# Attention and two dense layers on one core: TensorE's operations grouped by kind within a slot, and an order of their own for the first five slots

## The reference

```python
scores = scale * np.matmul(q, k.transpose(0, 1, 3, 2))     # q, k, v: 2 x 8 heads x 576 x 64
kth = np.partition(scores, -32, axis=-1)[..., -32:-31]
scores = np.where(scores >= kth, scores, -1e9)
attn = exp(scores - max) / (sum + 1e-9)
x = matmul(attn, v)                                        # as 1152 rows x 512
x = ((x @ w_a) * (x @ w_b)) @ w_out                        # 512 -> 1536 -> 512
p = domain_probs / (domain_probs.sum(-1) + 1e-9)
out = sum over e of p[:, e] * (relu(x @ w1[e]) @ w2[e])    # 4 experts, 512 -> 1024 -> 512
```

## Time and profile before

| | |
|---|---|
| time, median of 3 runs (lowest, highest) | 848.16 us (845.84, 848.91) |
| the profiled execution | 849.11 us, span 847.3 us |
| mean granted clock | 0.972 |
| busy: PE, PEld, DVE, ACT, POOL | 807.8, 713.1, 457.9, 384.6, 297.1 us |
| instructions | 13113 |

### The profile page before, as it was taken

How to read it: one execution, slowest core, us unless ns; L and a number is a source line. 1 busy time by engine, 2 the same in 40 slices (tenths; PEclk the granted TensorE clock), 3 DMA queues, 4 the chain that set the end, 5 groups by cost and what they waited for, 6 DMA issues and landing times.

```text
span 847.3 us, 13113 instructions
## 1 busy us (share of the span) xinstructions
PE 807.8 (95%) x4985; PEld 713.1 (84%) x4985; DVE 457.9 (54%) x902; ACT 384.6 (45%) x712; POOL 297.1 (35%) x269
## 2 busy tenths in 40 slices
PE   4468999999999999999999999999999999999998
PEld 3346788888888888888889899899899898898996
DVE  5979999899999999998124112122121121221121
ACT  5665787777777777777444011311032010230110
POOL 3766875454545454545331000530016000440000
PEclk9557999999999999999999999999999999999999
DMA  9540685456545654445688500230004100000000
GB/s 233 160 117 1 219 242 206 150 193 200 187 148 183 254 170 158 163 155 173 209 285 300 219 1 1 99 100 1 1 1 141 58 1 1 1 1 38 14 25 38
DMA packets 71631, 102.59 MB, mean 121 GB/s; under 512 B 32528, under 2 KB 48912, under 8 KB 71568
## 3 DMA queue, kind: packets, MB, share of 16 engines
q1 hardware_dynamic: 70512, 101.48, 36.6%
q10 hardware_dynamic: 1056, 0.26, 0.2%
HBM read 88.36 MB, written 13.37 MB: 120 GB/s over the span
## 4 chain that ended last, share of the span: by engine, by line
PE 88%; ACT 4%; POOL 4%; issue 2%; DMA 1%; DVE 1%; SPq 0%; ACTq 0%; POOLq 0%
PE ps L612 24%; PE ps L632 23%; PE ps L522 16%; PE ps L507 8%; PE ps L471 5%; PE ps L442 5%; PE ps L451 4%; PE ps L480 1%; POOL p_sb L1007 1%; ACT p_sb L702 1%; POOL wa_lo L1041 1%; DMA wo<-wo_d 1%; PE ps L402 1%; ACT pT L709 1%; PE ps L514 0%
## 5 line engine op out<-in xcount | busy, mean ns | idle before, releaser
L769 ACT ACTIVATE h_hi<-ps 128x384 fp32r<-128x384 f32 x96 | 47.0, 491 | 269.7 <-PE ps L612 269.5
L874 DVE MAX8 m<-work 128x8 f32<-128x576 f32 x216 | 152.3, 747 | 0.0
L1057 POOL TENSOR_TENSOR w_lo<-w_raw,w_hi 128x2048 fp32r<-128x2048 f32 x12 | 55.1, 4617 | 244.5 <-ACT w_hi L765 244.5
L933 DVE SCALAR_TENSOR_TENSOR h_lo<-ps,h_hi 128x384 fp32r<-128x384 f32 x96 | 53.3, 557 | 156.8 <-ACT h_hi L769 156.8
L612 PE MATMUL ps<-x_hi,w_hi 128*128 128x384 f32 x384 | 129.0, 336 | 0.0
L612 PE MATMUL ps<-x_hi,w_lo 128*128 128x384 f32 x384 | 128.8, 336 | 0.0
L612 PE MATMUL ps<-x_lo,w_hi 128*128 128x384 f32 x384 | 128.8, 335 | 0.0
L632 PE MATMUL ps<-w_hi,h_hi 128*128 128x512 f32 x288 | 112.2, 390 | 0.0
L632 PE MATMUL ps<-w_hi,h_lo 128*128 128x512 f32 x288 | 112.2, 390 | 0.0
L632 PE MATMUL ps<-w_lo,h_hi 128*128 128x512 f32 x288 | 112.1, 389 | 0.0
L880 DVE MATCH_REPLACE8 work<-m,work 128x576 f32<-128x576 f32 x144 | 106.0, 743 | 0.0
(11 more groups left out here) (90 smaller groups left out, 1507.8 us busy)
## 6 DMA issues: line engine op xcount, KB each, us to landing
wo<-wo_d SPq DMA_DIRECT2D x96, 512.0 KB, 4.9
w_raw<-moe_w_in SPq DMA_DIRECT2D x16, 1024.0 KB, 6.6
wo_d<-wo SPq DMA_DIRECT2D x12, 512.0 KB, 4.5
w_raw<-moe_w_a_in SPq DMA_DIRECT2D x4, 768.0 KB, 6.0
w_raw<-moe_w_b_in SPq DMA_DIRECT2D x4, 768.0 KB, 5.5
wo_raw<-moe_w_out_in SPq DMA_DIRECT2D x12, 256.0 KB, 3.9
v_sb<-v_in SPq DMA_DIRECT2D x18, 128.0 KB, 3.8
x_d<-x_hi_out SPq DMA_DIRECT2D x9, 256.0 KB, 3.0
```

What stands on the lines that cost most here:

```text
L769: copy(h_hi[:, m, :], ps[:, UP + m % FREE_UP, 0:GN], ACT.Relu).then_inc(ac_r, 1)
L874: nc.vector.max(m8[:, par, i, 8 * r:8 * r + 8], work[:, i, :]).then_inc(ve_top, 1)
L933: nc.vector.scalar_tensor_tensor(h_lo[:, m, :], ps[:, UP + m % FREE_UP, 0:GN], 0.0, h_hi[:, m, :].bitcast(F32), ALU.max, ALU.subtract).the ...
L1057: nc.gpsimd.tensor_tensor(lo[:, s, :], raw[s][:], hi[:, s, :].bitcast(F32), ALU.subtract).then_inc(done, 1)
```

## The change

TensorE's order in slots 5 to 40 becomes: scores, send, up(wa), y_transpose, h_transpose, p_transpose, up(wb), q_transpose, inv_spread, keys, weighted_sum. inv_transpose stands between the two heads of p_transpose and writes a part of bank 3 instead of ps_a; the waits on `ac_a` and `ac_i` that went with ps_a go. Slots 0 to 4 have a function `first_slot`: p_transpose, q_transpose, scores of pair n + 2, weighted_sum, inv_spread. (The scores of pair 1 are still made in slot 0, and slot 4 makes none.)

ScalarE: x_hi moves between the two below_tops, y_out between the two exponentials, and p_out with inv_turned moves from behind the copy of a to ahead of slice_hi and chunk_hi. VectorE: sums after 1 pass instead of 2; for tile 0, sums after pass 10 of pair 4 (was 8), scale and x_low after passes 2 and 4 of pair 5 (were 4 and 6).

```diff
--- before.py
+++ after.py
@@ -443,8 +443,11 @@
                                                   kT[rows, b, pr, cols], start=True, stop=True)
                 mm.then_inc(pe_s, 1)
 
-            def p_transpose(n):
+            def p_transpose(n, t):
                 for head in range(2):
+                    if head and t is not None:
+                        pe.wait_ge(ac_s, 2 * min(n + 2, NP - 1) + head + 1)
+                        inv_transpose(t)
                     pe.wait_ge(ac_e, 2 * n + head + 1)
                     pe.wait_ge(ac_s, 2 * min(n + 2, NP - 1) + head + 1)
                     for c in range(KC):
@@ -482,7 +485,7 @@
 
             def inv_transpose(t):
                 pe.wait_ge(ve_den, 2 * t + 2)
-                nc.tensor.transpose(ps_a[:, 0:P], x_inv[:].rearrange("p r h -> p (r h)"), ident[:]).then_inc(pe_i, 1)
+                nc.tensor.transpose(ps[:, 3, P:2 * P], x_inv[:].rearrange("p r h -> p (r h)"), ident[:]).then_inc(pe_i, 1)
 
             def inv_spread(t):
                 pe.wait_ge(ac_i, 2 * t + 1)
@@ -536,7 +539,25 @@
             q_transpose(range(1, PR), ps_x)
             for pr in range(1, PR):
                 keys_pair(0, pr)
-            for n in range(LAST + 1):
+            def first_slot(n):
+                if n == 0:
+                    scores(1)
+                else:
+                    p_transpose(n - 1, scaled_tile(n + 1))
+                if next_q(n) is not None:
+                    pe.wait_ge(ld_q, 16 + 32 * next_q(n))
+                    q_transpose(range(PR), ps_a)
+                if n < LAG_AB - 1:
+                    scores(n + 2)
+                if n:
+                    weighted_sum(n - 1)
+                if scaled_tile(n + 1) is not None:
+                    pe.wait_ge(po_pick, PR + 1)
+                    inv_spread(scaled_tile(n + 1))
+
+            for n in range(LAG_AB):
+                first_slot(n)
+            for n in range(LAG_AB, LAST + 1):
                 m, u = unit_of(n), turned_unit(n)
                 if scaled_tile(n) is not None:
                     pe.wait_ge(ac_i, 2 * scaled_tile(n) + 2)
@@ -546,41 +567,30 @@
                     scores(n + 1)
                 if sent_of(n) is not None:
                     send(sent_of(n))
+                if m < PR:
+                    pe.wait_ge(po_w, SLICES.index((0, m)) + 1)
+                if m % PR == 0:
+                    pe.wait_ge(ve_xT, m // PR + 1)
+                pe.wait_ge(ac_a, m)
+                pe.wait_ge(ac_q, min((n + 1) // PR + 2, NT + 1))
+                up(wa_hi, wa_lo, ps_a, m, pe_a)
+                if finished_tile(n) is not None:
+                    y_transpose(finished_tile(n))
                 if u is not None:
                     h_transpose(u)
-                if m is not None:
-                    if m < PR:
-                        pe.wait_ge(po_w, SLICES.index((0, m)) + 1)
-                    if m % PR == 0:
-                        pe.wait_ge(ve_xT, m // PR + 1)
-                    pe.wait_ge(ac_a, m)
-                    if n % PR == 1:
-                        pe.wait_ge(ac_i, 2 * min(n // PR, NT))
-                    pe.wait_ge(ac_q, min((n + 1) // PR + 2, NT + 1))
-                    up(wa_hi, wa_lo, ps_a, m, pe_a)
-                if finished_tile(n) is not None:
-                    y_transpose(finished_tile(n))
                 if pair_of(n) is not None:
-                    p_transpose(pair_of(n))
-                if scaled_tile(n + 1) is not None:
-                    if m is not None:
-                        pe.wait_ge(ac_a, m + 1)
-                    inv_transpose(scaled_tile(n + 1))
-                if m is not None:
-                    if m < PR:
-                        pe.wait_ge(po_w, SLICES.index((1, m)) + 1)
-                    pe.wait_ge(ac_b, m)
-                    if u is not None:
-                        pe.wait_ge(ac_h, 2 * u + 2)
-                    up(wb_hi, wb_lo, ps_b, m, pe_b)
+                    p_transpose(pair_of(n), scaled_tile(n + 1))
+                if m < PR:
+                    pe.wait_ge(po_w, SLICES.index((1, m)) + 1)
+                pe.wait_ge(ac_b, m)
+                if u is not None:
+                    pe.wait_ge(ac_h, 2 * u + 2)
+                up(wb_hi, wb_lo, ps_b, m, pe_b)
                 if next_q(n) is not None:
-                    if m is not None:
-                        pe.wait_ge(ac_a, m + 1)
+                    pe.wait_ge(ac_a, m + 1)
                     pe.wait_ge(ld_q, 16 + 32 * next_q(n))
                     q_transpose(range(PR), ps_a)
                 if scaled_tile(n + 1) is not None:
-                    if n == PR:
-                        pe.wait_ge(po_pick, PR + 1)
                     pe.wait_ge(ac_pT, 2 * pair_of(n) + 2)
                     inv_spread(scaled_tile(n + 1))
                 if n in KEYS1:
@@ -711,7 +721,7 @@
 
             def inv_turned(t):
                 act.wait_ge(pe_i, 2 * t + 1)
-                copy(invT[:], ps_a[:, 0:P], ACT.Copy).then_inc(ac_i, 1)
+                copy(invT[:], ps[:, 3, P:2 * P], ACT.Copy).then_inc(ac_i, 1)
 
             def inv_out(t):
                 act.wait_ge(pe_i, 2 * t + 2)
@@ -783,24 +793,30 @@
                 j, m, u = pair_of(n), unit_of(n), turned_unit(n)
                 if j is not None:
                     below_top(j, 0)
+                if scaled_tile(n) is not None:
+                    x_hi(scaled_tile(n))
+                if j is not None:
                     below_top(j, 1)
                 if n + 1 < NP:
                     scores_out(n + 1, 0)
-                if scaled_tile(n) is not None:
-                    x_hi(scaled_tile(n))
                 if j is not None:
                     exponentials(j, 0)
+                if finished_tile(n) is not None:
+                    y_out(finished_tile(n))
+                if j is not None:
                     exponentials(j, 1)
                 if n + 1 < NP:
                     scores_out(n + 1, 1)
-                if finished_tile(n) is not None:
-                    y_out(finished_tile(n))
                 if u is not None:
                     h_out(u)
                 if n in (NP + 2, NP + 3):
                     act.wait_ge(pe_x, NP)
                     act.wait_ge(pe_s, NP)
                     expert_hi(0, n - NP - 2, 0)
+                if j is not None:
+                    p_out(j)
+                if scaled_tile(n + 1) is not None:
+                    inv_turned(scaled_tile(n + 1))
                 for i in HIGH_IN.get(n, ()):
                     slice_hi(i)
                 for g in CHUNKS_IN.get(n, ()):
@@ -809,10 +825,6 @@
                     act.wait_ge(pe_a, m + 1)
                     act.wait_ge(po_h, m)
                     copy(a_sb[:], ps_a[:, 0:FS], ACT.Copy).then_inc(ac_a, 1)
-                if j is not None:
-                    p_out(j)
-                if scaled_tile(n + 1) is not None:
-                    inv_turned(scaled_tile(n + 1))
                 if finished_tile(n) is not None:
                     x2_out(finished_tile(n))
                 if m is not None:
@@ -862,7 +874,7 @@
                 for i in range(2):
                     dve.wait_ge(ac_s, 2 * n + i + 1)
                     nc.vector.max(m8[:, par, i, 0:8], s_sb[:, ring[i], :]).then_inc(ve_top, 1)
-                between(n, 2)
+                    between(n, 1 + i)
                 for i in range(2):
                     dve.wait_ge(ve_top, base + i + 1)
                     nc.vector.match_replace(work[:, i, :], m8[:, par, i, 0:8], s_sb[:, ring[i], :], LOWEST).then_inc(ve_top, 1)
@@ -907,8 +919,8 @@
                 nc.vector.tensor_tensor(xT_lo[:, t % 2, :, :], xu[:].rearrange("p (c t) -> p c t", c=DK),
                                         xT_hi[:, t % 2, :, :].bitcast(F32), ALU.subtract).then_inc(ve_xT, 1)
 
-            SUMS, SCALE, LOW = 2, 10, 11
-            FIRST_SUMS, FIRST_SCALE, FIRST_LOW = 8, 4, 6
+            SUMS, SCALE, LOW = 1, 10, 11
+            FIRST_SUMS, FIRST_SCALE, FIRST_LOW = 10, 2, 4
 
             def between(n, done):
                 t = scaled_tile(n)
```

## The result

The changed kernel takes 856.85 us (median of 4 runs, 856.14 to 857.28), the kernel before 847.25 in the same comparison (845.84 to 848.91): ratio 1.0121, 95% interval 1.0100 to 1.0141. It is 9.6 us slower. The profiled execution took 857.28 us with a span of 855.5, 8.2 more than the one of before. The other 1.4 us are spread between executions: the profiled one of before lay 1.9 us above its median in this comparison, the one of after 0.4 above. What follows accounts for the 8.2.

The account below looks back on a forecast made before the run. TensorE bounds the kernel from slot 5 on, a ring of waits before. Front -2.5, full slots +2.2 and tail +5.2 give +4.9 us on 848.2, 853.1, taken as 852.8 for the clock; range 845.5 to 857.

Parts of the forecast that it names:

- 7.0 us at up(wa) in slot 5: First five slots: with scores two slots ahead, up(wa) starts at 64.4 us, 7.0 us earlier.
- -2.9 in slot 5 and -0.7 in each of slots 6 to 9: p_out ahead of slice_hi and chunk_hi delays GpSimd: 2.9 us given back in slot 5, 0.7 in each of four slots.
- +1.2 given back from x_hi and y_out: Slots 9 and 10: tile 1's x_hi leaves the gap (0.5 us), y_transpose no longer follows the last y_out (some 0.7).
- The wait of up(wb) for h_out: Slots 10 to 36: up(wb) waits for h's copies, 0.11 to 0.16 us in 20 slots without inv_transpose, 2.9 us.
- Fewer changes between transposes and products: Slots 10 to 36: h_transpose's move saves one change a slot, 0.5 us over 27 slots, at most 2.4.
- The xT wait that goes: Full slots: the xT wait in seven scaled slots, 0.1 us each, goes, saving 0.7 us.
- Slot 35: In slot 35 x2_out and with it push_down come later, costing 0.5 us.
- Tail: Slots 37 to 40: four 1.2 us idles of up(wb) and 2.0 us for a late w_out reload, +5.2 us in all.
- The front was not kept whole: Rival: GpSimd's late pieces gate nothing, TensorE keeps 7.0 us, 848.6 us; chance 0.23, 0.12 of it with smaller waits.
- No DMA wait in the tail: Rival: the x2 store comes in time, tail +3.2 instead of +5.2 us, 850.8 us; chance 0.18.
- The grouping: Rival: 0.09 us per saved change and a hidden h_out wait, full slots -1.0 instead of +2.2, 849.6 us; chance 0.08.
- The clock did not fall in the full slots: Rival: the clock falls in longer transpose blocks, 19 us over ten y_transpose slots, 870 us or more; chance 0.02.

Follow-up runs that it names:

- both_back: The changed kernel with h_transpose back ahead of up(wa) and p_out with inv_turned back behind the copy of a: 841.53 us, ratio 0.9931 to before.
- no_first_slot: both_back with the first five slots in an order like that of before, scores one slot ahead: 841.68 us, ratio 0.9931 to before.
- front_only: both_back with x_hi behind the first scores_out and y_out behind the second again: 847.25 us, ratio 1.0002 to before.
- pout_back: The changed kernel with p_out and inv_turned back behind the copy of a in ScalarE's order: 852.39 us, ratio 1.0059 to before.
- h_back: The changed kernel with h_transpose back ahead of up(wa) in every slot: 847.32 us, ratio 1.0002 to before.
- h_copy_short: The changed kernel with hT_raw copied for one of three chunks only, from unit 1 on: 851.26 us, ratio 1.0044 to before.

## Why the prediction was right in its direction and short in its size

Slower was right, and so were the two mechanisms of loss: p_out ahead of the weights' high parts, and up(wb) waiting for h's copies. The median of 856.85 lies just inside the range. The forecast was 852.8, a loss of 4.6 us where 9.6 were measured. The sum was +4.9, and the traces have +8.2. Two terms of it were mis-sized, the front by 1.8 us and the full slots by 1.6; what the front's gain comes from was also wrong. The 0.3 us taken off for the clock did not come, and 1.4 us are the spread of the profiled executions.

**Front: forecast 2.5 us ahead, measured 0.7.** The steps of it:

- *7.0 us at up(wa) in slot 5.* Measured 6.1 there, and 6.9 in slot 10 without either of the moves that cost (both_back). But I put nearly all of it to the scores. VectorE's idle of 4.46 us did go (sums at 55.14, forecast 55.2), yet that was worth little: no_first_slot and front_only give 1.5 us at the most to the scores and 5.5 to the places of x_hi and y_out (no run parts these two; it is x_hi that x_low waits for), whose part in slot 5 I had not looked at. So the 7.0 was near 6.9 in part by luck. I had read the 2.70 us of x_low as a risk for the new order, when it was a cost of the old one: here x_low took 0.68 us; it began just as one push_down ended (64.50 against 64.49), which nothing in my working had placed there.
- *-2.9 in slot 5 and -0.7 in each of slots 6 to 9, 5.7 together.* Measured 5.0 (pout_back), in the two halves 2.9 and 2.3. The mechanism was right: product(0) at 77.09 (forecast 76.3), GpSimd waiting for wb_hi. Not in it were the fall of the clock at 80.7 us and, in slot 9, the held x_low.
- *h_transpose's move.* I counted it from slot 10 on. It costs 1.25 us in slots 6 to 10 as well (pout_back against both_back, 127.11 against 125.86), or 0.9 with p_out early (the changed kernel against h_back).
- *+1.2 given back from x_hi and y_out.* It did not come: in slot 9 up(wa) waited 1.29 us for x_low of tile 1, which it does not in before, and in slot 10 y_transpose waited 1.04 us for its own copy xu, 0.27 in before. With p_out back neither wait is there.

6.9 - 5.0 - 1.25 leaves the 0.7 us of the trace. The three are the steps from before over both_back and pout_back to the changed kernel, so they add up by construction.

**Full slots: forecast +2.2, measured +3.8.** Term by term:

- *The wait of up(wb) for h_out, forecast 2.9.* Measured 4.2 (285.52 against 281.36 in h_back). It is some 0.19 us in each slot without inv_transpose, and 0.07 to 0.11 in the seven with it, where I had said that one transpose more covers it. The uncovered time was right at 1.34 us (1.45 with inv_transpose); the release took 1.55 (1.90 in slot 35), instead of 1.45 to 1.50. A difference of two lengths of 1.4 us each was too fine for the rows that I took them from.
- *Fewer changes between transposes and products, forecast -0.5.* Measured nothing (h_copy_short against h_back).
- *The xT wait that goes, forecast -0.7.* Measured -0.7 (front_only against both_back, 281.67 and 281.01).
- *Slot 35, forecast +0.5.* That slot is 0.4 us longer than before, and so it is in h_back; it is not in both_back. It goes with p_out's move.

**Tail: forecast +5.2, measured +5.0, with another make-up.** The idle of 1.2 us is there four times (1.05). The wait for a DMA of w_out in slot 40 is not. In its place the send of slot 39 waits for x2_out behind expert_hi; that expert_hi pushes x2_out back was in the forecast, and that send restarts ps_y and needs x2_out itself was not. The forecast's own terms (4.8 - 0.65 - 0.3 + 2.0) add up to 5.85, not 5.2; the 5.2 came from lengths of 19.8 and 23.8 us for slots 38 to 40, where the traces have 21.7 and 25.2 from send to send. So that this term came out within 0.2 us is luck. The two waits hide each other in part: without the first the second is 2.05 us, and both moved away give 4.3 of the 5.0.

**The rivals.** The front was not kept whole; it needed 5 us and kept 0.7. "No DMA wait in the tail" was right in its word and wrong in its time, for the reason above. The grouping does not pay: with the h_out wait gone and the blocks kept (h_copy_short) it gives nothing. The clock did not fall in the full slots. In the table of stretches it is 1.00 from 110 us on with blocks of up to 17 transposes. Its one fall after slot 5 began, at 80.7 us, came behind 2.32 us in which TensorE stood idle, and not in pout_back, which has the same blocks and where it stood idle for 0.49 us there. The idle time alone doesn't settle it: in h_back 2.57 us of it, ahead of h_transpose at 77.62, were followed by no fall. By the Trainium skill, TensorE: Matmul & The Clock Gate, Part 4: PE-mode transpose, transposes do not count as busy in the way products do; no effect of that shows with these blocks.

**The profile's signs.** Seen as forecast: VectorE's idle ahead of sums gone, up(wa) near 64 us (65.28), the last wb_lo waiting for wb_hi, up(wb) waiting for hT_raw, 1.05 us in the last four slots. Not seen: the longer wait of send for w_out.

Open are the 0.7 us of the tail that neither edit of it removes, and what makes the executions of before spread (845.2 to 849.8 in one comparison, where no_first_slot has 841.3 to 843.0).

## What to carry to other kernels

- A producer moved close to its consumer exposes the copy between them. Ask what work stands between the producer and the first instruction that overwrites its bank; here 2.1 us of products had covered a 1.55 us round over ScalarE, and 1.34 us of transposes do not. In the slots without transposes nothing does.
- A change of several moves can hold a gain and a loss of the same size: this one gains 6.9 us in its first ten slots and loses more than twice that in two moves that can be undone alone (841.53 against 856.85). Undo one move at a time, and look at each section's length, not at the end alone.
- If an engine's order is changed, look at each longer operation that stands behind the moved one on the other engines (here slice_hi, chunk_hi, expert_hi), and at who waits for the one behind that.

## What the runs showed of the hardware

A VectorE subtraction with both inputs in SBUF takes 0.68 us, and in these traces it does not run side by side with a subtraction of GpSimd's: the one that starts second ends later. In the trace of before x_low ran from 68.57 to 71.27; GpSimd's timeline of before has

```profile
67.28 3.44 POOL L1041 TENSOR_TENSOR wa_lo<-w_raw,wa_hi 128x1536 fp32r<-128x1536 f32 x1
```

which ends at 70.72. In front_only GpSimd's ends at 69.53 and x_low at 70.08. Both times x_low ends 0.55 us behind GpSimd's operation, whenever it began: 2.70 and 3.86 us. The same in slot 9 of the changed kernel, under a push_down that ends at 115.43:

```profile
114.44 1.54 DVE L919 TENSOR_TENSOR xT_lo<-xu,xT_hi 128x512 fp32r<-128x512 f32 x1 [0.52 <-ACT xT_hi L735]
```

The other way round it is GpSimd that takes longer. In both_back the first push_down ended at 64.72, x_low ran its 0.68 us from 64.73 to 65.41, and the second push_down, which began at 64.77, took 1.92 us where the first had taken 1.42:

```profile
64.77 1.92 POOL L1019 TENSOR_TENSOR p_sb<-s_sb,p_sb 128x576 f32<-128x576 f32 x1
```

The Trainium skill, GPSIMD Engine Reference, 1. Specifications, says that GpSimd shares its SBUF interfaces with VectorE, with contention for VectorE's instructions that have two SBUF inputs. The traces agree.
